# First MLP weights loaded between head pairs and split by ScalarE and VectorE inside attention, in a fused attention, MLP and mixture-of-experts kernel

## The reference

```python
# attention: q, k, v are 2 x 8 heads x 768 x 64; n_sink = 4, window = 128
keep = (pos[None, :] < n_sink) | ((rel >= 0) & (rel < window))
a = softmax(where(keep, q @ k.T / sqrt(64), -1e9)); attn = a @ v
x = attn as 1536 tokens x 512
# MLP: w_in 512 x 2048, w_out 2048 x 512
h = x @ w_in; r = maximum(h, 0); x = (r * r) @ w_out
# mixture of 8 experts, top 2 of noisy router logits, w1 512 x 1024, w2 1024 x 512
out[token] += weight * (maximum(x @ w1[e], 0) @ w2[e])
```

## Time and profile before

| what | us |
|---|---|
| median of 3 runs | 782.74 (781.65 to 784.48) |
| the profiled execution, its own time | 783.07 |
| its span in the profile | 781.3 |
| TensorE busy in the span | 731.9 (94%) |
| VectorE, ScalarE, GpSimd busy | 321.1, 279.3, 112.6 |

### The profile page before, as it was taken

The page is one execution under the profiler, slowest core; times in us unless marked ns, Lnnn a source line. Parts: engine busy times, 40 slices in busy tenths (PEclk is TensorE's granted clock), DMA queues, the critical chain, the costliest instruction groups (busy, mean ns, idle before and its releaser), DMA issues.

```text
span 781.3 us, 12123 instructions
## 1 busy us (share of the span) xinstructions
PE 731.9 (94%) x4844; PEld 619.1 (79%) x4844; DVE 321.1 (41%) x728; ACT 279.3 (36%) x533; POOL 112.6 (14%) x99
## 2 busy tenths in 40 slices
PE   5588998999999999999998999999999999999992
PEld 4477876888778888888887889898988888898981
DVE  5487872542221532225654173524343433425200
ACT  4455762431232322223432163425242333434210
POOL 5291000000000040000503210201111020202011
PEclk9888998999999999999999999999999999999997
DMA  7954628920000020004434517382817355372122
GB/s 231 333 156 131 213 72 317 372 90 1 0 1 1 2 108 3 0 0 170 155 134 179 151 35 262 41 284 28 268 43 195 124 130 187 60 266 31 24 28 29
DMA packets 40282, 94.80 MB, mean 121 GB/s; under 512 B 6176, under 2 KB 6176, under 8 KB 40224
## 3 DMA queue, kind: packets, MB, share of 16 engines
q1 hardware_dynamic: 33696, 79.17, 29.1%
q0 software_dynamic: 6528, 14.83, 9.6%
HBM read 68.24 MB, written 25.75 MB: 120 GB/s over the span
## 4 chain that ended last, share of the span: by engine, by line
PE 87%; DVE 4%; DMA 3%; ACT 3%; issue 1%; SPq 0%; POOL 0%; DVEq 0%; ACTq 0%; POOLq 0%
PE ps L1384 22%; PE ps L1369 21%; PE ps L1296 17%; PE ps L1286 16%; PE ps L1211 2%; PE ps L1179 2%; PE ps L1357 2%; DMA k_sb<-kT 2%; ACT s_probs L569 1%; PE ps L1192 1%; DVE s_inv L803 1%; PE ps L1193 1%; PE ps L1313 1%; DVE s_probs L790 1%; PE ps L1307 1%
## 5 line engine op out<-in xcount | busy, mean ns | idle before, releaser
L1384 PE MATMUL ps<-w_hi,hT_hi 128*128 128x512 f32 x256 | 102.8, 401 | 0.0
L1384 PE MATMUL ps<-w_hi,hT_lo 128*128 128x512 f32 x256 | 100.4, 392 | 0.0
L1384 PE MATMUL ps<-w_lo,hT_hi 128*128 128x512 f32 x256 | 100.0, 391 | 0.0
L1023 DVE TENSOR_TENSOR w_lo<-w_raw,w_hi 128x2048 fp32r<-128x2048 f32 x36 | 82.6, 2294 | 37.0 <-ACT w_hi L648 37.0
L526 POOL DMA_INDIRECT out<-y_sb,meta_tok x32 | 50.5, 1578 | 286.5 <-DVE meta_w L1066 139.4
L1074 DVE SCALAR_TENSOR_TENSOR hT_lo<-ps,hT_hi 128x448 fp32r<-128x448 f32 (+2 forms) x64 | 39.8, 624 | 122.9 <-ACT hT_hi L686 122.8
L907 DVE SCALAR_TENSOR_TENSOR g_sb<-ps,g_sb 128x512 f32<-128x512 f32 x48 | 33.2, 692 | 120.1 <-ACT g_sb L614 118.9
L614 ACT ACTIVATE g_sb<-ps 128x512 f32<-128x512 f32 x48 | 28.7, 598 | 143.3 <-PE ps L1286 143.3
L686 ACT ACTIVATE hT_hi<-ps 128x448 fp32r<-128x448 f32 (+2 forms) x64 | 34.7, 544 | 123.8 <-PE ps L1369 123.8
L1296 PE MATMUL ps<-w_hi,gT_hi 128*128 128x512 f32 x192 | 76.6, 399 | 0.5 <-DVE gT_lo L909 0.3
L515 POOL DMA_INDIRECT expert_rows<-x_rows,slots_i x24 | 26.8, 1117 | 344.4 <-DVE slots_i L1013 338.0
(11 more groups left out here) (161 smaller groups left out, 1168.2 us busy)
## 6 DMA issues: line engine op xcount, KB each, us to landing
w_raw<-w SPq DMA_DIRECT2D x32, 1024.0 KB, 9.2
xg<-expert_rows SPq DMA_DIRECT2D x32, 262.0 KB, 11.1
v_sb<-v SPq DMA_DIRECT2D x8, 832.0 KB, 4.6
expert_rows<-pad_rows SPq DMA_DIRECT2D x24, 262.0 KB, 3.8
w_raw<-w_in SPq DMA_DIRECT2D x4, 1024.0 KB, 8.5
w_raw<-w_out SPq DMA_DIRECT2D x4, 1024.0 KB, 12.7
vt_sb<-v_tail SPq DMA_DIRECT2D x8, 480.0 KB, 7.1
k_sb<-kT SPq DMA_DIRECT2D x8, 456.0 KB, 8.0
```

What stands on the lines that cost most here:

```text
L1023: dve.tensor_tensor(piece(w_lo, s, i), piece(w_raw, s, i), piece(w_hi, s, i).bitcast(F32), ALU.subtract).then_inc(ready, 1)
L1384: m = pe.matmul(ps[:, Y_BANKS[t % 2], :], a[:, f, rows_of(t)], w[:, slot, l2_cols(f)], start=(f == 0 and k == 0), stop=(f == HALF_F - 1 an ...
```

## The change

- SyncE no longer issues slot 0's loads before the choice of the path. In the short path it issues pieces 0 and 1 behind the loads of pair 2, and pieces 2 and 3 behind those of pair 3. Each piece has its own semaphore.
- GpSimd splits nothing of slot 0 any more.
- Pieces 0 and 1 are cut into 16 parts of 128x256. In iterations 7 to 22 ScalarE makes the `hi` of one part behind the high part of x (`first_hi`), and VectorE its `lo` behind the low part of x (`first_lo`).
- Pieces 2 and 3 are split whole, on ScalarE (`second_hi`) and VectorE (`second_lo`), after attention and ahead of the first MLP step.
- TensorE does layer 1 of the first step inside attention: behind the output of batch 23 and ahead of the turns of batches 22 and 23. It waits only for the x of batches 0 to 11, which is all that the first group of tokens needs. `attn_done` is awaited by TensorE only after the first group.
- Layer 2 of the first group waits for pieces 2 and 3 by themselves.
- On all engines the general path stands ahead of the short path in the program. The jump over it is now taken before attention and not after it.

```diff
+        SMALL = 2 * PIECE // 16
+        SPLIT_FROM = BATCHES - 16 - 1
@@ SyncE
-            for i in range(4):
-                sp.dma_start(piece(w_raw, 0, i), mlp_source(0, i)).then_inc(mlp_w_in, 16)
+            def load_first(i):
+                sp.dma_start(piece(w_raw, 0, i), mlp_source(0, i)).then_inc(mlp_w_in[i], 16)
...
+                    load_v(pair, pair % 2)
+                    if pair < 4:
+                        load_first(2 * pair - 4)
+                        load_first(2 * pair - 3)
@@ GpSimd
-            pool.wait_ge(mlp_w_in, 16 * 4)
-            for i in range(4):
-                split(0, i, mlp_w_split)
@@ ScalarE
+            def first_hi(k):
+                act.wait_ge(mlp_w_in[k // 8], 16)
+                act.activation(small(w_hi, k), small(w_raw, k), ACT.Copy).then_inc(first_hi_done, 1)
+            def second_hi(i):
+                act.wait_ge(mlp_w_in[i], 16)
+                act.activation(piece(w_hi, 0, i), piece(w_raw, 0, i), ACT.Copy).then_inc(first_hi_done, 1)
...
                     if n >= 1:
                         s_high(n - 1)
+                    if 0 <= n - SPLIT_FROM < 16:
+                        first_hi(n - SPLIT_FROM)
                 s_high(BATCHES - 1)
...
+            for i in range(2, 4):
+                second_hi(i)
@@ VectorE
+            def first_lo(k):
+                dve.wait_ge(first_hi_done, k + 1)
+                dve.tensor_tensor(small(w_lo, k), small(w_raw, k), small(w_hi, k).bitcast(F32), ALU.subtract).then_inc(mlp_w_split, 1)
+            def second_lo(i):
+                dve.wait_ge(first_hi_done, 16 + i - 1)
+                dve.tensor_tensor(piece(w_lo, 0, i), piece(w_raw, 0, i), piece(w_hi, 0, i).bitcast(F32),
+                                  ALU.subtract).then_inc(mlp_w_split, 1)
...
+                    if n >= 1:
+                        s_low(n - 1)
+                    if 0 <= n - SPLIT_FROM < 16:
+                        first_lo(n - SPLIT_FROM)
...
+            for i in range(2, 4):
+                second_lo(i)
 
             dve.wait_ge(router_in, 48)
             mlp_group(0, True)
@@ TensorE
+                    s_output(n)
+                    if n == BATCHES - 1:
+                        pe.wait_ge(x_lo_done, PB * DC)
+                        layer1(0, 0, True)
+                    if n >= 1:
+                        s_turn(n - 1)
+                s_turn(BATCHES - 1)
...
-                    pe.wait_ge(mlp_w_split, 4 * (s + 1))
+                    pe.wait_ge(mlp_w_split, 16 + 6 * s)
...
+            def layer2(g, f, first):
...
+                if first and f in (0, HALF_F // 2):
+                    pe.wait_ge(mlp_w_split, 17 + f // (HALF_F // 2))
...
+            mlp_group(0, True)
+            pe.wait_ge(attn_done, 1)
             pe.wait_ge(router_in, 48)
-            mlp_group(0, True)
```

More of the change, by code:

```diff
@@ L875, in _ @@
             with dve.If(short == 0):
+              for k in range(16):
+                  first_lo(k)
               dve.wait_ge(iota_done, 1)
@@ L896, in _ @@
               dve.sem_inc(attn_done, 1)
+            with dve.If(short == 1):
+                s_mask(0)
+                s_mask(1)
+                s_copy_tail(0)
+                s_invert(0)
+                for n in range(BATCHES):
+                    if n + 2 < BATCHES:
+                        s_mask(n + 2)
+                    if n + 1 < BATCHES:
+                        s_copy_tail(n + 1)
+                        s_invert(n + 1)
+                    s_norm(n)
+                    if n >= 1:
+                        s_low(n - 1)
+                    if 0 <= n - SPLIT_FROM < 16:
+                        first_lo(n - SPLIT_FROM)
+                s_low(BATCHES - 1)
+                dve.wait_ge(x_lo_done, BATCHES)
+                dve.sem_inc(attn_done, 1)
             dve.wait_ge(consts_done, 1)
@@ L1225, in s_turn, with layer1 @@
                 t.then_inc(s_oT, 1)
+            def layer1(g, f, first):
+                b = f % 2
+                s, fl = f // HALF_F, f % HALF_F
+                n = FC1 * g + f
+                if first and fl == 0:
+                    pe.wait_ge(mlp_w_split, 16 + 6 * s)
+                if not (first and f < 2):
+                    pe.wait_ge(m_sq, n - 1)
+                for i, (w, x) in enumerate(((w_hi, xT_hi), (w_hi, xT_lo), (w_lo, xT_hi))):
+                    for c in range(DC):
+                        m = pe.matmul(ps[:, 4 + b, :], w[:, s, l1_cols(c, fl * P, P)], x[:, c, bass.ds(g * GROUP, GROUP)],
+                                      start=(i == 0 and c == 0), stop=(i == 2 and c == DC - 1))
+                m.then_inc(m_l1, 1)
             pe.wait_ge(short_ready, 1)
             short = pe.value_load(is_short[:, :], min_val=0, max_val=1)
-            with pe.If(short == 1):
-                s_score(0)
-                s_score(1)
-                pe.wait_ge(consts_done, 1)
-                s_transpose(0)
-                for n in range(BATCHES):
-                    if n + 2 < BATCHES:
-                        s_score(n + 2)
-                    if n + 1 < BATCHES:
-                        s_transpose(n + 1)
-                    s_output(n)
-                    if n >= 1:
-                        s_turn(n - 1)
-                s_turn(BATCHES - 1)
             with pe.If(short == 0):
@@ L1325, in mlp_group @@
                 for f in range(FC1):
-                    layer1(g, f, first)
+                    if not (first and f == 0):
+                        layer1(g, f, first)
                     if f >= 1:
@@ L1331, in mlp_group @@
                             pe.wait_ge(y_dve, 2 * g)
-                        layer2(g, f - 1)
+                        layer2(g, f - 1, first)
                     if not first:
```

91 lines of the change are left out of this document (36 added, 55 removed).

## The result

The changed kernel takes **786.38 us** (median of 12 runs, 784.93 to 790.64) against 782.54 for the kernel before on the same chip (12 runs, 780.81 to 785.39): a ratio of 1.0048, 95% interval 1.0031 to 1.0064. It is slower by half a per cent where 772.9 was forecast. The profiled execution took 786.11, its span is 784.3; before it was 783.07 and 781.3.

A forecast was written before the change was run, and what follows sets the result against it. TensorE was taken to bound the kernel, so the change's worth lay in when the MLP's steady matmuls begin. Terms -19.6 + 4.8 + 0.5 + 1.9 + 2.6 = -9.8 us gave 772.9 us, range 769.0 to 778.5 (8 in 10).

The forecast's parts named there:

- Part 3: Jump over the general path, now ahead of attention: +0.5 us, bounds 0 and 4.2.
- own signs of being wrong: In attention: k of pair 3 ends a TensorE wait, first mask after 13, or masks stay 3.48 us apart with parts.
- part 4: Start of the MLP, batch 23's output to layer 2: 16.2 us instead of 14.31, +1.9, with two whole pieces split there.
- The rival of 776.6: At the start, VectorE's first mask waits for instruction fetch while DMA queues are full, costing 4.2 us; chance 0.20.
- estimate of no stall: Jump ahead of attention: 176 rows to jump, by the skill's rule of two held 256-instruction blocks, give no stall.
- Part 1: Inside attention: moving slot 0's loads and removing GpSimd's split wins back the 19.6 us lost there, -19.6.
- The rival that GpSimd isn't the cause: In attention, VectorE's two stalls of 3.7 us stay, giving 780.3 us; chance 0.05.
- The estimate for k: In attention, pair 3's k lands at about 38.0, needed at 39.5 for batch 9's scores, so fits by 1.5 us.
- The slower rival of one such stall: In attention, weights hold back k once, costing what pair 2's did: 783.9 us; chance 0.01 for a single late k.
- Part 2: 16 weight parts in attention's ring: 14 masks delayed by 0.34 us each, +4.8 us (4.0 to 7.0).
- the mask rows: VectorE rows in attention, 0.38 long and begun 0.30 apart, cited for a part's smaller step in the ring.
- Part 5: TensorE's clock falls during its wait before the MLP's layer 2, restarting at half clock: +2.6 us, bounds 0 and 3.2.

The follow-up runs named there:

- ladder 1: Changed kernel with the short path first on all engines, as it was before: 777.64 us, ratio 0.9914.
- ladder 3: ladder 1 with one weight piece a pair, first_lo ahead of the low part of x, and parts begun one iteration earlier: 774.87 us, ratio 0.9892.
- before_general_first: Kernel before with only the order of the two paths changed, general path first on TensorE, VectorE, ScalarE and SyncE: 785.33 us, ratio 1.0017.
- Ladder 4: ladder 3 with piece 3 split in MLP step 1, no longer ahead of step 0: 772.45 us, ratio 0.9846; run again 771.59 us, ratio 0.9833.
- pe_short_first: Changed kernel with only TensorE's two paths put back to short path first: 782.44 us, ratio 0.9997.
- halves_spread: Ladder 4 with pieces loaded behind the next pair's q and k, in halves, each half at its own batch: 769.48 us, ratio 0.9820.
- qk_ahead: Ladder 4 with each weight piece issued behind the next pair's q and k instead of ahead of them: 771.63 us, ratio 0.9831.

## Why the prediction was wrong

**Part 3, the jump, is the step that failed.** The prediction took 0.5 us, with bounds 0 and 4.2, and said that "TensorE's and ScalarE's jumps hide under the wait for k until 8.2 and for the mask until 12". Measured by the mask of batch 5, the start lost 9.5 us, 9.0 more than the term. The order of the paths alone brings this loss into the kernel before (9.0 at batch 4), and putting it back takes it away (ladder 1). Two of the prediction's own signs of being wrong came: the first mask at 17.58, after 13, and a wait that k of pair 3 ended. Three things were wrong in the term. TensorE's jump does not run beside the wait for k: it is taken at 8.2, when VectorE's value is there, and lasts 7.0 us from then on. Behind it TensorE stood for another 2.17 us in straight code, which the term does not have. And the jump's price was bounded by VectorE's gap after attention, where the DMA engines had less to do; at the start it was 5.7 us for VectorE, above the upper bound. The view of the branch's own line in the trace before would have given 3.36 us for TensorE; the issue wait of 3.13 in the earlier trace rows, which part 4 counted only as something that goes away, was this same jump. The rival of 776.6 had the mechanism, code fetched while the DMA queues are full, but put it on VectorE alone and at less than half its size.

The Trainium skill (Runtime: NRT & Kernel Launch, section on instruction fetch) says that a taken branch stalls only where its target is outside the two blocks of 256 instructions at hand. By that rule the prediction made an estimate of no stall for 176 rows. VectorE's jump of 2.9 us with idle DMA engines and 5.7 with full ones says otherwise: here the measurement decides. Whether the rule or the estimate failed stays open. No row here gives the 176. By the Trainium skill's section a block of 256 instructions has 16 KiB, and that is the size of q8's packets (0.02 MB), but those of q14, on which VectorE's jumps end, are half as large (0.01 MB). The Trainium skill's section also says that straight code crosses a block at a cost that is mostly hidden; the waits of up to 2.53 us in ladder 3 differ from that where the DMA share is near 1.

**Part 1, -19.6.** The two causes were rightly named. In the changed kernel no four-column operation is held and the 8.35 us wait is gone. The rival that GpSimd isn't the cause falls: with its split gone there is no such stall, and in before_general_first, where the split no longer lies in the wait for k, there are four, each ending with a subtraction of GpSimd's. But "I cost the loads at nothing" was wrong: k of pairs 3 and 4 ended waits of 1.41 and 1.94 us, and with the batches at the lower clock behind the second the pace lost 4.3: the 71.2 us between the masks of batches 5 and 23 are 18 x 3.48 + 14 x 0.30 = 66.8 and the rest. The estimate for k was 38.0 against a need at 39.5. With the start 9.5 later, it was 50.48 against 49.07. The 12.7 us counted from the issue of v (34.84) would have ended at 47.5; k took 3 us longer. The sum left out that v and the pieces of pair 4 were issued from 45.27 on, while k was still on its way; that this made the 3 us was not tested by itself. The slower rival of one such stall (783.9) took the size of pair 2's stall; its direction was right.

**Part 2, +4.8.** Right: 14 parts at 0.30 are 4.2. The duration is 0.41 us, and only 0.30 of it are in the ring, as the mask rows said. The Trainium skill (VectorE: DVE Perf Modes, section on the TRN2 errata) is near with its 424 ns for the duration; its fixed latency is largely hidden behind the instruction ahead.

**Part 4, +1.9.** Right: 16.06 from output to layer 2, with 16.2 forecast. Two whole pieces ahead of the square are the last thing to end, as said. Ladder 4, which moves one of them, takes 14.97 where ladder 3 takes 17.03.

**Part 5, +2.6.** Right in kind, too large in size: layer 2 begins at half clock, and that costs 1.5 us. From the first matmul of layer 2 in step 0 to that in step 1 (134.71 before, 136.40 after) are 5.6 us before and 7.1 after:

```profile
134.71 0.40 PE L1296 MATMUL ps<-w_hi,gT_hi 128*128 128x512 f32 x1
136.40 0.40 PE L1334 MATMUL ps<-w_hi,gT_hi 128*128 128x512 f32 x1
```

The 2.6 came from a restart before that held half clock for some 5 us; this one holds it for about 3 (129.30 to 132.4). In pe_short_first, where the jump keeps TensorE from running ahead, the wait is 2.10 us instead of 7.52 and the first matmul takes 0.50 us, but the granted clock falls in the step itself (0.50 from 126 to 129 us), and from step to step it is 7.2.

**The sum again.** Against the forecast the start is 9.0 us more, k 4.3 more, the parts 0.6 less, the start of the MLP 0.1 less and the clock 1.1 less: -9.8 + 9.0 + 4.3 - 0.6 - 0.1 - 1.1 = +1.7 us. The spans differ by 3.0 and the medians by 3.8. Of the spans' difference 1.4 lie in the experts, which the change doesn't touch: from the last matmul of the MLP to the last of all are 362.2 us before and 363.6 after. Two executions of ladder 4, the same kernel, have 362.0 and 364.5 there, so this is scatter between executions.

## What to carry to other kernels

A taken branch is an operation with a price: look up the branch's own line in the trace, and the gap from it to the next instruction on the same engine, before you move one to a place where an engine is awaited. Here it cost 9.5 us ahead of the work. Behind attention it cost 1.2 us from output to layer 2 where other work ran beside it (ladder 1 against the changed kernel), and 4.4 in the kernel before, where it didn't (14.31 against 9.88, the restart at half clock included). Loads for later stages put into a tuned loop are not free: a long burst made k late, and with k ahead of it made TensorE's instructions late; short and spread loads left the least waits of all rungs of the ladder (1.71 us), though their gain in time is not clear of the noise. When a wait goes and the time stands still, look for new waits put down to issue, and for the instruction queue's packet ahead of them. And before a rest of a span is given to a cause, look where in the program it lies.

## What the runs showed of the hardware that I had not expected

- A jump over a path that isn't taken cost TensorE 7.0 us and VectorE 5.7 while the DMA share was near 1, 5.3 and 2.9 when the queues emptied during it, and ScalarE 0.5. Behind attention TensorE's was 3.36.
- Straight code of TensorE stood still for 0.30 to 2.53 us at fixed places of the program, with no semaphore to wait for, 34 times in these profiles, each time with the DMA share near 1 (0.89 or more) while the code was on its way. The same place gave 1.98 in two executions of one kernel, 1.71 with spread loads, and 0.61 with q and k ahead.
- TensorE went on 1.2 to 1.7 us behind the end of a packet of the instruction queue, in straight code and behind jumps alike. What the load of the DMA engines changed was the time until that packet started: 4.5 us behind the branch with full engines, 2.7 while they emptied, 1.0 behind attention.
- Layer 2 begins 16.1 us earlier in halves_spread than before (112.99 for 129.09), and the span is 13.3 shorter. Of the other 2.8, 0.4 lie in the first step of the MLP and 2.2 in the experts (364.4 for 362.2 us), within what two executions of ladder 4 differ by.
- The lowest median is that of halves_spread: 769.48 us, 0.982 of the kernel before; its interval overlaps those of ladder 4 and qk_ahead.
